# Routed experts: rows gathered by token, tags scattered, and each slot adding its own result to the output

## The reference, cut to what matters

```python
def reference(...):
    x = attention(q, k, v, a_re, a_im)        # rows of 384, 3072 tokens
    x = ln(solu(x @ w_in)) * g_ln @ w_out     # first feed-forward, 384 -> 1024 -> 384
    noisy = x @ w_gate + log1p(exp(x @ w_noise)) * noise
    top2, top2_w = the two largest of 8 experts, softmax over the two
    out = zeros((3072, 384))
    for e in range(8):
        for k in range(2):
            mask = top2[:, k] == e
            h = maximum(x[mask] @ w1[e], 0)
            out[mask] += top2_w[mask, k, None] * (h @ w2[e])
```

## Time and profile before

| | |
|---|---|
| median of 3 runs | 1532.5 us (1527.84 to 1536.19) |
| the profiled execution: its own time, its span | 1527.98 us, 1526.2 us |
| PE busy | 1177.6 us, 77% of the span |
| DVE busy | 938.0 us, 61% |
| ACT busy | 656.9 us, 43% |
| POOL busy | 263.2 us, 17% |
| mean rate of all transfers | 120 GB/s |

### The profile page before, as it was taken

How to read it: one execution, slowest core, us unless ns; L and a number is a source line. 1 busy time by engine, 2 the same in 40 slices (tenths; PEclk the granted TensorE clock), 3 DMA queues, 4 the chain that set the end, 5 groups by cost and what they waited for, 6 DMA issues and landing times. The chain is left out here.

```text
span 1526.2 us, 23562 instructions
## 1 busy us (share of the span) xinstructions
PE 1177.6 (77%) x8058; PEld 1009.5 (66%) x8058; DVE 938.0 (61%) x1912; ACT 656.9 (43%) x1022; POOL 263.2 (17%) x268
## 2 busy tenths in 40 slices
PE   0033868688997799799999369999999999999910
PEld 0022546466665566566667259999999999999900
DVE  5695399458965689635453356666666666666533
ACT  4312623463346433523333135555555555555400
POOL 3010503142232323213231100000000000000065
PEclk9966888798998999999999679999999999999965
DMA  8002001310022100211110276666566666665267
GB/s 240 8 16 94 16 16 32 106 53 26 27 58 92 42 27 32 65 32 37 43 42 12 95 256 211 227 229 222 208 225 227 206 209 225 230 223 208 102 174 208
DMA packets 86099, 183.10 MB, mean 120 GB/s; under 512 B 9648, under 2 KB 52912, under 8 KB 85264
## 3 DMA queue, kind: packets, MB, share of 16 engines
q1 hardware_dynamic: 75424, 151.17, 30.2%
q0 software_dynamic: 6144, 18.88, 4.1%
q10 hardware_dynamic: 4464, 12.19, 2.0%
HBM read 146.01 MB, written 32.64 MB: 117 GB/s over the span
## 5 line engine op out<-in xcount | busy, mean ns | idle before, releaser
L1312 PE MATMUL bank<-sxh,w1h 128*128 128x256 f32 x744 | 212.6, 286 | 1.9 <-DVE sxl L1265 1.9
L1312 PE MATMUL bank<-sxh,w1l 128*128 128x256 f32 x744 | 210.7, 283 | 0.0
L1312 PE MATMUL bank<-sxl,w1h 128*128 128x256 f32 x744 | 210.5, 283 | 0.0
L850 ACT ACTIVATE hh<-bank 128x256 fp32r<-128x256 f32 x248 | 95.2, 384 | 219.1 <-PE bank L1312 219.1
L1277 DVE SCALAR_TENSOR_TENSOR hl<-bank,hh 128x256 fp32r<-128x256 f32 x248 | 104.8, 423 | 131.0 <-ACT hh L850 130.9
L1486 PE MATMUL bank<-w2h,hh 128*128 128x384 f32 x496 | 170.4, 344 | 6.8 <-DVE hl L1277 2.9
L1486 PE MATMUL bank<-w2l,hh 128*128 128x384 f32 x496 | 166.9, 337 | 0.0
L1486 PE MATMUL bank<-w2h,hl 128*128 128x384 f32 x496 | 166.6, 336 | 0.0
L635 POOL DMA_INDIRECT ga<-ys,row_u x48 | 46.1, 960 | 606.9 <-DMA ys<-yo 592.6
L1254 DVE TENSOR_TENSOR w1l<-raw,w1h 128x1024 fp32r<-128x1024 f32 x93 | 113.9, 1226 | 53.2 <-ACT w1h L814 53.2
L1312 PEld LDWEIGHTS bank<-sxh,w1h 128*128 128x128 f32 x744 | 141.0, 190 | 2.3 <-DVE sxl L1265 2.3
(11 more groups left out here) (185 smaller groups left out, 2565.9 us busy)
## 6 DMA issues: line engine op xcount, KB each, us to landing
raw<-in_w SPq DMA_DIRECT2D x62, 1536.0 KB, 6.7
xg<-xs SPq DMA_DIRECT2D x31, 384.0 KB, 7.2
ys<-yo ACTq DMA_DIRECT2D x31, 384.0 KB, 6.4
qk<-in_q SPq DMA_DIRECT2D x48, 96.0 KB
qk<-in_k SPq DMA_DIRECT2D x48, 96.0 KB
vt<-in_v SPq DMA_DIRECT2D x24, 192.0 KB
out<-gc SPq DMA_DIRECT2D x24, 192.0 KB
ar<-in_a_re SPq DMA_DIRECT2D x3, 1152.0 KB, 5.3
```

What stands on the lines that cost most here:

```text
L850: nc.scalar.activation(hh[:, f % NH, :], bank[:, f % 2, 0:CAP], ACT.Relu).then_inc(hh_done, 1)
L1312: ins = MM(dst, stationary[a_](cc), moving[b_](cc), start=(n_ == 0), stop=(n_ == len(terms) - 1))
```

## The change

- `xs` holds each token's row once, in token order, written by SP with a plain transfer in the first phase (`send_rows`). The scatter on POOL writes 8 bytes for each routed row instead, a tag of token number and gate weight, into `tags`, which has the regions that `xs` had.
- The space behind each region's last row is filled with the tag of that expert's last row: DVE works out where it lies (`last_step`, 6 small operations), POOL reads 8 tags, DVE spreads them (`pad_tag`), SP writes them (8 transfers of 2 KB).
- For each slot SP loads the tags (`load_mine`, three buffers), POOL gathers the slot's rows from `xs` by token number (two indirect gathers of 128 rows) and the rows of `out` as they stand (`partial`, two more), DVE computes weight times result plus `prev` (`give`, two instructions, in the place of ACT's copy), and POOL scatters the two halves into `out`, the second after the first has landed.
- `ys`, the tail and its gathers go; the output is zeroed at the start (9 transfers). The loops over slots are written out.

```diff
 # SP
-            for j in range(PADS):
-                sp.dma_start(flat_rows(xs[at0:at0 + CAP]), wide[...]).then_inc(pad_sent, 16)
+            for at0 in range(0, T * DM, NP * 2 * P):
+                sp.dma_start(plain[:, at0:at0 + NP * 2 * P], wide[...]).then_inc(out_zeroed, 16)
...
+            def send_rows(par, j):
+                apart(sp, (x2_evac, j + 1))
+                sp.dma_start(xs[bass.ds(j * P, P)], x2[par][:]).then_inc(x_sent[par], 16)
...
-            def load_rows(s, par):
-                row = sp.value_load(slot_row[0:1, bass.ds(s, 1)], ...)
-                apart(sp, (sxt_mm, s - 1))
-                sp.dma_start(xg[par][:]..., flat_rows(xs[bass.ds(row, CAP)])).then_inc(xg_loaded[par], 16)
+            def load_mine(s, k):
+                row = sp.value_load(slot_row[0:1, bass.ds(s, 1)], ...)
+                apart(sp, (y_sent, 32 * (s - 2)))
+                sp.dma_start(mine[k][:]..., tags[bass.ds(row, CAP)]...).then_inc(mine_loaded[k], 16)
...
-                sp.dma_start(flat_rows(xs[bass.ds(row, CAP)]), zeros[:]).then_inc(pad_sent, 16)
+                sp.dma_start(tags[bass.ds(row, CAP)]..., pad_tag[e:e + 1]...).then_inc(pad_sent, 16)
+            sp.wait_ge(pad_sent, 16 * E)
             first_phase_over(sp)
-            load_rows(0, 0)
+            load_mine(0, 0)
             load_w2(0)
+            load_mine(1, 1)
-                if more:
-                    load_rows(s + 1, 1 - par)
-                    load_w1(s + 1)
-                    load_w2(s + 1)
+            for s in range(SLOTS - 1):
+                if s + 2 < SLOTS:
+                    load_mine(s + 2, (s + 2) % 3)
+                load_w1(s + 1)
+                load_w2(s + 1)
 # POOL
-                    apart(pool, (pos_step, 5 * g_ + 5), (x2_evac, g_ + 1))
+                    apart(pool, (pos_step, 5 * g_ + 5), (w_step, 3 * g_ + 3), (const_ready, 9))
                     for e in range(2):
-                        nc.gpsimd.indirect_dma_start(xs, ...idx..., x2[par][:], None)
+                        nc.gpsimd.indirect_dma_start(tags, ...idx..., tag[:, g_, e, :], None)
...
-            slots_over(pool)
-            for t in range(T):
-                for e in range(2):
-                    nc.gpsimd.indirect_dma_start(ga[t % NB][:, e, :], None, ys, ...row_u...)
+            def gather(s, par, k):
+                pool.wait_ge(mine_loaded[k], 16 * (s // 3 + 1))
+                wait(pool, sxt_mm, s - 1)
+                for u in range(SUB):
+                    nc.gpsimd.indirect_dma_start(xg[par][:, u, :], None, xs, ...mine[k][:, u, 0:1]...)
+            def partial(s, par, k):
+                wait(pool, y_sent, 32 * s)
+                wait(pool, y2_evac, 2 * (s - 1))
+                for u in range(SUB):
+                    nc.gpsimd.indirect_dma_start(prev[par][:, u, :], None, out, ...mine[k][:, u, 0:1]...)
+            def give(s, par, k):
+                pool.wait_ge(y2_evac, 2 * (s + 1))
+                for u in range(SUB):
+                    wait(pool, y_sent, 32 * s + 16 * u)
+                    nc.gpsimd.indirect_dma_start(out, ...mine[k][:, u, 0:1]..., yo[par][:, u, :], None).then_inc(y_sent, 16)
+            gather(0, 0, 0)
+            gather(1, 1, 1)
+            for s in range(SLOTS):
+                if 2 <= s + 1 < SLOTS:
+                    gather(s + 1, (s + 1) % 2, (s + 1) % 3)
+                partial(s, s % 2, s % 3)
+                give(s, s % 2, s % 3)
 # ACT
-                    if f == 0 and not first:
-                        give(s - 1, 1 - par, half if par else half - 1)
-                    if f == 1 and not first:
-                        send(s - 1, 1 - par)
 # DVE
+            def give(s, par, k):
+                dve.wait_ge(y2_mm, FC * (s + 1))
+                wait(dve, y_sent, 32 * (s - 1))
+                dve.wait_ge(mine_loaded[k], 16 * (s // 3 + 1))
+                dve.wait_ge(prev_loaded[par], 32 * (s // 2 + 1))
+                for u in range(SUB):
+                    V.scalar_tensor_tensor(out=yo[par][:, u, :], in0=bank[:, 2 + u, 0:DM], scalar=mine[k][:, u, 1:2]...,
+                                           in1=prev[par][:, u, :], op0=ALU.mult, op1=ALU.add).then_inc(y2_evac, 1)
...
                     ... hl of chunk f ...
+                    if f == 0 and s > 0:
+                        give(s - 1, 1 - par, (s - 1) % 3)
-            for t in range(T):
-                V.tensor_scalar(gb[t % NB][:], ga[t % NB][:, 0, :], gate_w[:, t, 0:1], None, ALU.mult)
-                V.scalar_tensor_tensor(out=gc[t % NB][:], in0=ga[t % NB][:, 1, :], scalar=gate_w[:, t, 1:2], ...)
 # PE
-                    wait(pe, y2_evac, s)
+                    wait(pe, y2_evac, 2 * s)
```

More of the change, by code:

```diff
@@ L195, in solu_moe_program @@
         yo = [m2(f"yo{i}", [P, SUB, DM]) for i in range(2)]
[L196 to L203, removed]
+        prev = [m2(f"prev{i}", [P, SUB, DM]) for i in range(2)]
+        mine = [m2(f"mine{i}", [P, SUB, 2], U32) for i in range(3)]
         bank = psum("bank", [P, 8, 512])
@@ L277, in solu_moe_program @@
         x_sent = [sem(f"x_sent{i}") for i in range(2)]
+        tag_sent = [sem(f"tag_sent{i}") for i in range(2)]
         slot_step = sem("slot_step")
-        zeros_ready = sem("zeros_ready")
+        out_zeroed = sem("out_zeroed")
+        idle_sent = sem("idle_sent")
+        last_step = sem("last_step")
+        last_loaded = sem("last_loaded")
         pad_sent = sem("pad_sent")
+        prev_loaded = [sem(f"prev_loaded{i}") for i in range(2)]
+        mine_loaded = [sem(f"mine_loaded{i}") for i in range(3)]
         raw1_loaded = sem("raw1_loaded")
@@ L296, in solu_moe_program @@
         y2_evac = sem("y2_evac")
[L297 to L301, removed]
+        y_sent = sem("y_sent")
         W2P = 4
@@ L365, in first_phase_over @@
             for s_ in x_sent:
+                eng.wait_ge(s_, 16 * T // 2)
+            for s_ in tag_sent:
                 eng.wait_ge(s_, 32 * T // 2)
-        def slots_over(eng):
-            for i in range(2):
-                eng.wait_ge(y_sent[i], 16 * len(range(i, SLOTS, 2)))
         @block.sync
@@ L462, in body @@
                     load_v(b, c, n)
+                if 0 <= n - 3 < T:
+                    send_rows((c + 1) % 2, n - 3)
                 if n == 1:
@@ L499, in _ @@
+            sp.wait_ge(pad_sent, 16 * E)
+            sp.wait_ge(idle_sent, 16)
             first_phase_over(sp)
[L500 to L501 removed]
+            load_mine(0, 0)
             load_w2(0)
[L504 to L513 removed]
@@ L514, in _ @@
-            for i in range(NB):
-                sp.wait_ge(out_sent[i], 16 * len(range(i, T, NB)))
+            load_mine(1, 1)
[4 more added lines that the diff above has]
+                load_w2(s + 1)
+            sp.wait_ge(out_zeroed, 16 * 9)
+            sp.wait_ge(y_sent, 32 * SLOTS)
         @block.gpsimd
@@ L831, in _, with slot @@
                 w2_piece(0, 0, j)
[L833 to L846, removed]
+            def slot(s, par, more):
                 for f in range(FC):
@@ L856, in slot @@
                         w2_piece(s + 1, 1 - par, f - 1 - KC)
-                    if f == 1 and not first:
-                        send(s - 1, 1 - par)
                     if more and f == FC - 4:
                         tokens(s + 1, 1 - par)
[L862 to L870, removed]
+            for s_ in range(SLOTS):
+                slot(s_, s_ % 2, s_ < SLOTS - 1)
         @block.vector
@@ L1237, in _ @@
             then(V.tensor_scalar(slot_expert[:], slot_f[:, 0, :], float(E - 1), None, ALU.min))
             then(V.tensor_copy(tail_row[:], rank_base[one]))
-            first_phase_over(dve)
[L1242 to L1245, removed]
-                                 region_at[:].unsqueeze(1).to_broadcast(by_row), ALU.is_ge))
@@ L1247, in _ @@
-            then(V.tensor_tensor(past[:], past[:], cnt[:, 3, 0:E - 1].unsqueeze(1).to_broadcast(by_row), ALU.mult))
-            then(V.tensor_reduce(shift[:, 0, :], past[:], AX.X, ALU.add))
-            then(V.tensor_tensor(shift[:, 1, :], shift[:, 0, :], rows_, ALU.add))
-            then(V.tensor_copy(row_u[:].rearrange("p t e -> p (t e)"), shift[:, 1, :]))
+            last = last_row[:, 0, :]
+            dve.wait_ge(const_ready, 9)
+            V.tensor_scalar(last, slots, -1.0, 0.0, ALU.add, ALU.max).then_inc(last_step, 1)
@@ new lines, in _ @@
+            dve.wait_ge(last_step, 1)
+            V.tensor_scalar(last_row[:, 1, :], expert_no[:], float(REGION), None, ALU.mult).then_inc(last_step, 1)
+            dve.wait_ge(last_step, 2)
+            V.scalar_tensor_tensor(out=last_row[:, 2, :], in0=last, scalar=float(CAP), in1=last_row[:, 1, :], op0=ALU.mult,
+                                   op1=ALU.add).then_inc(last_step, 1)
+            dve.wait_ge(last_step, 3)
+            V.tensor_tensor(last, last_row[:, 2, :], ident[:, 0:E], ALU.mult).then_inc(last_step, 1)
@@ L1285, in slot @@
                         tokens(s + 1, 1 - par)
```

(11 more changed lines are left out.)

99 lines of the change are left out of this document (61 added, 38 removed).

## The result

The changed kernel takes 1959.4 us (median of 4 runs, 1949.8 to 1966.2) against 1531.2 us (4 runs), a ratio of 1.279 with a 95% interval of 1.271 to 1.286. The forecast was 1905 us, 1790 to 2120. The profiled execution has a span of 1962.9 us (its own time 1964.8) against 1526.2 us.

What follows compares the result with a forecast made beforehand. PE was taken to set the pace in the slots, about 18.0 us each. From the profiled 1528.0: + 437 (28 stalled slots) + 2 (gap) + 1 (last slots) − 63 (tail) = 1905 us, range 1790 to 2120.

Steps and rivals of the forecast that it cites:

- The mechanism: Slots: SP's load_mine waits for slot s-1's scatters ahead of the weight loads, so ACT and PE stall in 28 slots, 437 us.
- the loads in time: Slots: weight loads arrive without a stall, so the tail's gain stands and the total is 1480 us; chance 0.04.
- the slow scatters: Slots: each scatter takes 6.4 us instead of 2.7, adding 7.4 a slot, total 2112 us; chance 0.09.
- the clock that stays down: Slots: PE's work behind the stall takes twice as long, 10.1 us more a slot, total 2188 us; chance 0.05.
- The repeated rows: Padded slots: transfers repeating one row take 6.4 us each, 52 us over 7 slots, total 1957 us; chance 0.04.
- The size of a stalled slot: Each of 28 slots grows by 13.3 us of waiting plus 2.3 of slow clock, 15.6 us.
- the signs: Expected in the profile after: ACT waiting about 12 us for w1 in 28 slots, slots of 33 to 34 us, a 10 us tail.
- The clock: Slots: after each stall PE restarts at 1.2 instead of 2.4 GHz for some 4.6 us, losing 2.3 us (1 to 5).
- Slots 29 and 30: Last two slots: only DVE's 1.25 us against ACT's 0.81 at the boundary, together 1 us.
- The tail: Behind the last product: 72.4 us shrink to 9.5, saving 63 us.
- The gap ahead of the slots: Between first phase and slots: added tag work and transfers mostly hidden, 2 us more, between 0 and 6.
- Phase one at 0: First phase: zeroing the output, tag scatters and send_rows cost nothing, covered by POOL's idle time; 0 us.

Runs made afterwards that it cites:

- the spare products: Changed kernel with 64 unread products on PE at f = 2 of slots 2 to 29: 1943.4 us; with 80 such products: 1912.8 us.
- the two edits together: Changed kernel with SP's weight loads ahead of load_mine and POOL's gather of slot s+2's rows ahead of slot s's scatters: 1504.0 us, 0.983 times before.

## Why the prediction was right, point by point

- **The mechanism held at each step.** ACT's wait for w1 comes 28 times, PE stands at the result of chunk 2, SP asks for w1 8.3 us behind the boundary in the slot shown and 8.6 on average. Two different edits that let w1 in ahead of `y_sent`, a new order and a fourth buffer, took 207 and 213 us away. Of the rivals, the loads in time, the slow scatters (2.85 us, not 6.4) and the clock that stays down (0.50 gives way to 1.00 within the slot, below) are out. The repeated rows are there at a sixth of their price: four padded slots were 2.3 us longer, 9 us in all instead of 52, and through a slower w1 load rather than slow scatters (3.1 to 3.2 us to land instead of 2.6).
- **The size of a stalled slot.** It was forecast as 15.6 and measured as 34.8 − 18.0 = 16.8. The steps to the issue of w1 took 0.8 less than the sum in the slot shown. The term that was too small is the landing of w1: 7.1 taken, 8.5 measured. That price came from w2 loads beside two plain transfers of 384 KB, the next rows and `ys`; here four gathers of 192 KB are issued within 5 us around the w1 load, and with two of them moved away the landing was 7.5. Averaged over the 28 slots, w1 is issued 8.6 us behind the boundary instead of 9.1 and lands 8.8 later instead of 7.1. That is 1.2 us a slot, and 28 × 1.2 = 34 us is all that the 471 lie above the forecast's 437. The padded slots' 9 us are part of it.
- **Two numbers of the working don't follow from its own terms.** From the bounds that it names (scatters of 2.3 to 3.0, landing of 6.6 to 9.1) a slot's low and high are 12.0 and 15.9, not 11.8 and 17.5, and the sums 1832 and 2053. And w1 at 16.2 with ACT ready 1.5 behind the boundary makes a wait of 14.7 for ACT, not the 12 among the signs; 446 / 28 = 15.9 was measured.
- **The clock.** PE took its work up again at 1338.96. The windows around it, columns as in the earlier trace rows:

```profile
1324.70:1338.80 14.10, 0.60 (x6) 0.39 (x4) 1.46 (x2) 2.54 (x5) 3.85 (x4) 0.69 0.83 285
...
1340.00:1342.00 2.00, 2.00 (x9) 1.90 (x9) 1.50 (x3) 0.00 (x0) 0.00 (x0) 0.50 0.00 0
1342.00:1344.00 2.00, 2.00 (x13) 2.00 (x12) 0.00 (x0) 0.00 (x0) 0.00 (x0) 0.60 0.00 0
1344.00:1346.00 2.00, 2.00 (x17) 2.00 (x16) 1.12 (x2) 1.82 (x3) 0.00 (x0) 1.00 0.00 0
```

  It stays at 0.50 through 1340 to 1342 and averages 0.60 in 1342 to 1344: some 4.6 us at 1.2 GHz, as in the one start of the earlier trace rows. The Trainium skill ("TensorE: Matmul & The Clock Gate", HAM oscillation) has each stalled tile start cold; the trace agrees in this slot, and the spare products put the price at 2.0 to 2.1 us.
- **Slots 29 and 30 were missed.** The forecast counted 1 us and the stretch took 8.7. Behind the boundary into slot 29, where w1 is already there:

```profile
1908.92 0.98 POOL L652 DMA_INDIRECT out<-yo,mine  x1 [25.62 <-DVE yo L1290]
...
1914.58 0.97 POOL L652 DMA_INDIRECT out<-yo,mine  x1 [4.67 <-DMA out<-yo,mine]
...
1917.15 0.97 POOL L632 DMA_INDIRECT xg<-xs,mine  x1 [0.30 <-issue]
...
1920.98 0.71 PEld L1319 LDWEIGHTS bank<-ident,xg 128*128 128x128 f32 x4 [6.89 <-DMA xg<-xs,mine]
```

  The gather of slot 30's rows is issued behind both scatters, and the first of these runs beside the w2 load (5.66 us to the next issue). PE waits 6.6 us for it. The sentence that "the gathers of rows ... all fit in the stall" was right for 28 slots, and this is what lay under the stall: a second wait of 6.5 us, which with its clock makes a slot 9 us longer. It was not priced as the rest that stays when the first is mended, and the rival with 1480 us assumed that nothing does.
- **The tail.** 59.7 of 63 saved:

```profile
1950.22 1.14 DVE L1290 SCALAR_TENSOR_TENSOR yo<-bank,mine,prev 128x384 f32<-128x384 f32 x2 [1.42 <-PE bank L1504]
1951.64 0.98 POOL L652 DMA_INDIRECT out<-yo,mine  x1 [7.35 <-DVE yo L1290]
1955.07 0.97 POOL L652 DMA_INDIRECT out<-yo,mine  x1 [2.44 <-DMA out<-yo,mine]
```

  The first of the last two scatters, of a slot that holds only one repeated row, takes 3.43 us to the next issue, 0.6 more than the 2.85 of a full one, and 7.8 us follow the second issue, where 4.5 were counted.
- **The gap ahead of the slots** grew by 4.9, inside 0 to 6 and above the 2 taken.
- **Phase one at 0** can't be refuted: +11.7 in the two profiles, but the kernel before differs from itself by 15.8 there.

## What to carry to other kernels

A wait costs most through what stands behind it in its queue. Before a load is put behind a semaphore, ask when the semaphore comes in the consumer's time and which statement follows: here 2 KB of tags, needed a slot later, held 3 MB of weights, half of which ACT was ready for 1.5 us into the slot. When a stall that costs 17 us a slot hides a second worth 9, mending the first gives only half; run the two edits together before judging the idea, since the idea itself (no tail) was worth 1.7%.

## What the runs showed of the hardware

- An indirect scatter of 128 rows of 1536 bytes into DRAM took 2.85 us from issue to the next issue behind its semaphore with no other transfer under way, 5.6 us beside a 1.5 MB load, and 3.4 us where the rows were one and the same.
- A 1.5 MB load landed after 8.5 us (median) with four indirect gathers of 192 KB issued around it, and after 7.5 or 7.6 with two of the four moved away, whichever two.
- Gathers that read one row again and again beside a load: with all reads of `out` turned into such, slots took 1.0 us more on average. The four padded slots took 2.3 us more, and lost this when the gather moved behind the load; why they cost more than the others stays open.
- The point at which the first phase ends moved between 853.1 and 875.6 us over executions of nearly the same instructions, and by 15.8 us between two of one kernel. A difference of 10 us there says nothing from one profile.
